# Prologue and first two slots of an attention and two-layer MLP kernel, each engine's calls written out one by one, without filler matmuls

## The reference, cut to what matters

```
q_d, k_d, v_d = mean of q, k, v over groups of 4 positions     # batch 4, heads 8, 576 positions, head dim 64
out_d   = softmax(q_d k_d^T / 8) v_d                           # 144 x 144 per head
out_up  = repeat(out_d, 4)
local   = softmax(where(|i - j| < 4, q k^T / 8, -1e9)) v
x  = (out_up + local), 2304 tokens x 512
x  = (max(x @ w_in1, 0)) ** 2 @ w_out1                         # 512 -> 2048 -> 512
x  = softplus(x @ w_in2) @ w_out2
```

## Time and profile before

| | us |
|---|---|
| median of 3 runs | 907.18 |
| the runs | 907.07, 907.18, 908.58 |
| profiled execution, its own time | 908.52 |
| its span, first to last instruction | 906.7 |
| TensorE busy | 887.1 (98%) |
| VectorE, ScalarE, GpSimd busy | 612.5, 440.0, 331.4 |
| granted clock of TensorE, mean | 0.992 |

### The profile page before, as it was taken

The page is one execution under the profiler, slowest core; times in us unless marked ns, Lnnn a source line. Parts: engine busy times, 40 slices in busy tenths (PEclk is TensorE's granted clock), DMA queues, the critical chain, the costliest instruction groups (busy, mean ns, idle before and its releaser), DMA issues.

```text
span 906.7 us, 14878 instructions
## 1 busy us (share of the span) xinstructions
PE 887.1 (98%) x5765; PEld 831.7 (92%) x5765; DVE 612.5 (68%) x1058; ACT 440.0 (49%) x1073; POOL 331.4 (37%) x160
## 2 busy tenths in 40 slices
PE   9889899999999999999999999999999999999998
PEld 7678799999999999999999998999989999899997
DVE  3779767866765776645145977767767777677675
ACT  4766354544546445453466634434444434434433
POOL 8699868688585976856100000000000000000000
PEclk9899999999999999999999999999999999999999
DMA  9770231221424221100145300200200200200000
GB/s 300 258 288 25 70 137 60 86 98 65 151 71 137 85 71 42 45 27 1 57 153 168 118 1 1 70 1 1 70 1 1 71 0 1 70 1 1 36 1 35
DMA packets 22037, 65.14 MB, mean 72 GB/s; under 512 B 2272, under 2 KB 9440, under 8 KB 21968
## 3 DMA queue, kind: packets, MB, share of 16 engines
q1 hardware_dynamic: 21968, 64.20, 21.0%
HBM read 54.76 MB, written 9.44 MB: 71 GB/s over the span
## 4 chain that ended last, share of the span: by engine, by line
PE 88%; POOL 6%; issue 2%; DVE 2%; ACT 1%; DMA 0%; POOLq 0%; DVEq 0%
PE bank L1285 22%; PE bank L1299 22%; PE bank L696 20%; PE bank L647 20%; POOL w_lo L725 2%; POOL prod L451 2%; POOL prod L405 1%; PE bank L545 1%; PE bank L288 1%; PE bank L590 1%; PE bank L472 1%; PE bank L615 1%; DMA qk_first<-in_qk_grp 0%; DVE xs L482 0%; ACT bank L565 0%
## 5 line engine op out<-in xcount | busy, mean ns | idle before, releaser
L647 PE MATMUL bank<-x_hi,w_hi 128*128 128x288 f32 x508 | 155.9, 307 | 3.9 <-DVE g_lo L685 2.1
L451 POOL TENSOR_TENSOR prod<-sc,vt 128x1344 f32<-128x1344 f32 x42 | 134.9, 3233 | 61.0 <-DVE sc L439 53.5
L685 DVE TENSOR_TENSOR g_lo<-bank,g_hi 128x288 fp32r<-128x288 f32 x128 | 58.4, 456 | 144.0 <-ACT g_hi L680 143.9
L696 PE MATMUL bank<-g_hi,w_hi 128*128 128x288 f32 x512 | 151.3, 295 | 0.0
L696 PE MATMUL bank<-g_hi,w_lo 128*128 128x288 f32 x512 | 151.1, 295 | 0.0
L696 PE MATMUL bank<-g_lo,w_hi 128*128 128x288 f32 x512 | 151.0, 295 | 0.0
L647 PE MATMUL bank<-x_lo,w_hi 128*128 128x288 f32 x508 | 150.9, 297 | 0.0
L647 PE MATMUL bank<-x_hi,w_lo 128*128 128x288 f32 x508 | 150.8, 297 | 0.0
L1011 ACT ACTIVATE sp_abs<-bank 128x384 f32<-128x384 f32 x96 | 47.0, 490 | 194.4 <-PE bank L1285 194.3
L405 POOL TENSOR_TENSOR prod<-qt,kt 128x1344 f32<-128x1344 f32 x42 | 133.1, 3175 | 17.9 <-DVE sc L412 12.3
L1285 PE MATMUL bank<-x_lo,w_hi 128*128 128x384 f32 x384 | 129.9, 338 | 0.0
(11 more groups left out here) (110 smaller groups left out, 1620.3 us busy)
## 6 DMA issues: line engine op xcount, KB each, us to landing
w_raw<-in_w SPq DMA_DIRECT2D x32, 512.0 KB, 4.8
qk<-in_qk_grp SPq DMA_DIRECT2D x12, 576.0 KB, 4.9
kt<-in_k_loc SPq DMA_DIRECT2D x7, 960.0 KB, 4.9
vt<-in_v_loc SPq DMA_DIRECT2D x7, 960.0 KB, 4.8
vg<-in_v_grp SPq DMA_DIRECT2D x16, 320.0 KB, 3.5
x_scratch<-ys SPq DMA_DIRECT2D x32, 144.0 KB, 3.2
x_raw<-x_scratch SPq DMA_DIRECT2D x6, 768.0 KB, 4.6
out<-y SPq DMA_DIRECT2D x18, 256.0 KB, 2.0
```

What stands on the lines that cost most here:

```text
L451: nc.gpsimd.tensor_tensor(dst, pb, win, ALU.mult).then_inc(prod_ready[m % 2], 1)
L647: last = nc.tensor.matmul(h_ps[f % 2][:, 0:NT], w[:, f, wc], x[:, T % 2, kc], start=(kc == 0 and i == 0), stop=(kc == KC - 1 and i == 2))
L685: nc.vector.tensor_tensor(g_lo[:, f % 2], h_ps[f % 2][:, 0:NT], g_hi[:, f % 2].bitcast(F32), ALU.subtract).then_inc(g_ready, 1)
L696: last = nc.tensor.matmul(y_ps[d][:, 0:NT], w[:, f, wc], g[:, f % 2], start=(f == 0 and i == 0), stop=(f == FC - 1 and i == 2))
```

## The change

It replaces the prologue's lists and the loops over slots 0 and 1 by lists of single calls, for all five queues. The calls are the same, with these exceptions and moves:

- all `keep_busy` calls are gone (the helper is redefined and no longer called; `first_x` loses its argument);
- SyncE: `first_load(1)` goes to second place, `v0` from second place to after `w_raw` 0 and slot 1's q and k; `w_raw` 0 goes ahead of slot 1's q and k; later loads are interleaved with the pair loads otherwise;
- GpSimd: the pools are interleaved otherwise, `weight_lo(0)` stands before the first `score_mult`, `first_pool_v(3)` after the third;
- ScalarE: `weight_hi(0)` after `first_exp(1)`, `weight_hi(1)` before `first_split_hi(1)`; `pair_exp` waits for `up_ready` for odd n above 4;
- VectorE: `score_sum(1, 0)` and `(1, 1)` before the last `first_split_lo`, `(1, 3)` before slot 0; in the slots the order is new throughout;
- TensorE: `pair_turn(0)` before `first_scores(2)`, `first_hidden_in` 0 and 1 before `first_x(2)`, and the attention's calls at other steps;
- waits on `mask_done` in `first_pool` and `first_pool_v`, since the mask is now a helper of its own (`local_mask`, the same calls, at the same place in the list).

The core of the diff (indentation cut by eight; slot 1, where the order of the same calls changes likewise, and what stood in the loops is left out):

```diff
     pool.wait_ge(first_qk[j], 16)
     if j:
         pool.wait_ge(qk0_pooled, j)
+        pool.wait_ge(mask_done, 1)
     two = qk_first[:, j].rearrange("p s (g f) -> p (s g) f", f=2)
     half = pairs0[:].rearrange("p s g -> p (s g)")
     nc.gpsimd.tensor_tensor(half, two[:, :, 0], two[:, :, 1], ALU.add).then_inc(pairs0_ready, 1)
...
 def first_pool_v(pool, j):
     pool.wait_ge(first_vg[j], 16)
+    pool.wait_ge(mask_done, 1)
     if j:
         pool.wait_ge(v0_pooled, j)
     two = vg0[0:GH, j].rearrange("g m (t f) -> g (m t) f", f=2)
...
 def keep_busy(pe, times):
     for _ in range(times):
-        nc.tensor.matmul(X0[:, 0:P], ident[:], ident[:], start=True, stop=True)
+        nc.tensor.matmul(t_ps[P - 32:P, 0:P], ident[:, P - 32:P], ident[:], start=True, stop=True)
 def first_scores(pe, j):
     pe.wait_ge(first_qk[j], 16)
...
     for e in range(2):
         nc.vector.tensor_copy(pT0[0:BK, j % 2, e], first_banks(j)[e][0:BK, 0:NT]).then_inc(pT0_copied, 1)
-def first_x(pe, j, busy):
+def first_x(pe, j):
     if j:
         pe.wait_ge(x0_ready, j)
         pe.wait_ge(up_ready, j)
-    keep_busy(pe, busy)
     if j == 0:
         pe.wait_ge(v0_loaded, 16)
     pe.wait_ge(pT0_copied, 2 * j + 2)
...
     a.wait_ge(ds_max, 2 * n + 2)
     if n:
         a.wait_ge(dp_ready, 2 * n)
+    if n > KC and n % 2:
+        a.wait_ge(up_ready, n)
     nc.scalar.activation(dnb[:], dmx[:], ACT.Copy, scale=-SCALE / (FACTOR * FACTOR)).then_inc(dnb_ready, 1)
     a.wait_ge(dnb_ready, n + 1)
     for e in range(2):
...
     def load_x2(i):
         sp.dma_start(x2_raw[:], x2_dram[:, :, i * NT2:i * NT2 + NT2]).then_inc(x2_loaded, 16)
+    def first_load_v0():
+        sp.dma_start(v0[0:BKR], v_first).then_inc(v0_loaded, 16)
+    def first_room_free():
+        sp.wait_ge(x0_ready, KC)
+        sp.wait_ge(up_ready, KC)
     first_load(0)
-    sp.dma_start(v0[0:BKR], v_first).then_inc(v0_loaded, 16)
+    first_load(1)
     first_load_v(0)
-    first_load(1)
     first_load(2)
+    first_load(3)
     first_load_v(1)
-    first_load(3)
     first_load_v(2)
+    weight_load(sp, 0, w1)
+    local_load_qk(1)
+    first_load_v0()
+    weight_load(sp, 1, w1)
+    weight_load(sp, 2, w1)
+    weight_load(sp, 3, w1)
+    weight_load(sp, 4, w1)
     first_load_v(3)
-    local_load_qk(1)
-    for f in range(3):
-        weight_load(sp, f, w1)
-    pair_load_qk(KC)
-    pair_load_v(KC)
-    for f in range(3, 5):
-        weight_load(sp, f, w1)
+    pair_load_qk(4)
+    weight_load(sp, 5, w1)
+    weight_load(sp, 6, w1)
+    weight_load(sp, 7, w1)
+    pair_load_v(4)
     local_load_v(1)
-    for f in range(5, LATE):
-        weight_load(sp, f, w1)
     pair_load_qk(5)
+    weight_load(sp, 8, w1)
+    first_room_free()
+    weight_load(sp, 9, w1)
+    weight_load(sp, 10, w1)
+    weight_load(sp, 11, w1)
+    weight_load(sp, 12, w1)
+    pair_load_qk(6)
+    weight_load(sp, 13, w1)
     pair_load_v(5)
-    sp.wait_ge(x0_ready, KC)
-    sp.wait_ge(up_ready, KC)
-    for f in range(LATE, FC):
-        weight_load(sp, f, w1)
-    pair_load_qk(6)
+    weight_load(sp, 14, w1)
     local_load_qk(2)
     pair_load_v(6)
+    weight_load(sp, 15, w1)
     local_load_v(2)
+    output_store(0)
     pair_load_qk(7)
-    for T in range(1, TILES):
+    pair_load_v(7)
+    local_load_qk(3)
+    pair_load_qk(8)
+    pair_load_v(8)
+    pair_load_qk(9)
+    local_load_v(3)
+    for T in range(2, TILES):
         C, A_next = 2 * T + 5, 2 * T + 6
-        if T == 1:
-            output_store(0)
+        if A_next < KC * B:
+            pair_load_qk(A_next)
+        if C < KC * B:
             pair_load_v(C)
-            pair_load_qk(A_next)
-            local_load_qk(3)
-        else:
-            if A_next < KC * B:
-                pair_load_qk(A_next)
-            if C < KC * B:
-                pair_load_v(C)
-            if T == TILES - 1:
-                sp.wait_ge(x_ready, KC * (TILES - 1))
-                sp.wait_ge(ys_stored, 16 * KC * (TILES - 2))
-                load_x2(0)
-            output_store(T - 1)
+        if T == TILES - 1:
+            sp.wait_ge(x_ready, KC * (TILES - 1))
+            sp.wait_ge(ys_stored, 16 * KC * 2)
+            load_x2(0)
+        output_store(T - 1)
         if T == 2:
             local_load_qk(4)
         if A_next < KC * B:
...
+    local_mask(pool)
     first_pool(pool, 1)
     first_pool_v(pool, 0)
+    first_pool(pool, 2)
     first_pool_v(pool, 1)
-    first_pool(pool, 2)
+    first_pool(pool, 3)
+    weight_lo(pool, 0, 0, w_lo_pool)
     first_pool_v(pool, 2)
-    first_pool_v(pool, 3)
-    first_pool(pool, 3)
     score_mult(pool, 1, 0)
     score_mult(pool, 1, 1)
-    def lo(f):
-        weight_lo(pool, f, 0, w_lo_pool)
-    lo(0)
-    lo(1)
     score_mult(pool, 1, 2)
-    lo(2)
+    first_pool_v(pool, 3)
     score_mult(pool, 1, 3)
-    lo(3)
+    weight_lo(pool, 1, 0, w_lo_pool)
+    weight_lo(pool, 2, 0, w_lo_pool)
+    weight_lo(pool, 3, 0, w_lo_pool)
     score_mult(pool, 1, 4)
-    lo(5)
     score_mult(pool, 1, 5)
-    lo(7)
-    lo(9)
+    weight_lo(pool, 5, 0, w_lo_pool)
+    weight_lo(pool, 7, 0, w_lo_pool)
+    weight_lo(pool, 9, 0, w_lo_pool)
     value_mult(pool, 1, 0)
     value_mult(pool, 1, 1)
-    lo(11)
+    weight_lo(pool, 11, 0, w_lo_pool)
     value_mult(pool, 1, 2)
     value_mult(pool, 1, 3)
-    lo(13)
     value_mult(pool, 1, 4)
+    weight_lo(pool, 13, 0, w_lo_pool)
     value_mult(pool, 1, 5)
-    lo(15)
-    for T in range(TILES - 1):
-        x_at = min(2 * T + 2, NPROD) if T < 2 else 5 if T == 2 else NPROD
+    weight_lo(pool, 15, 0, w_lo_pool)
+    score_mult(pool, 2, 0)
+    score_mult(pool, 2, 1)
+    x_split_lo(pool, 1)
+    score_mult(pool, 2, 2)
+    score_mult(pool, 2, 3)
+    score_mult(pool, 2, 4)
+    score_mult(pool, 2, 5)
+    value_mult(pool, 2, 0)
+    value_mult(pool, 2, 1)
+    value_mult(pool, 2, 2)
+    value_mult(pool, 2, 3)
+    value_mult(pool, 2, 4)
+    value_mult(pool, 2, 5)
+    score_mult(pool, 3, 0)
+    score_mult(pool, 3, 1)
+    score_mult(pool, 3, 2)
+    score_mult(pool, 3, 3)
+    x_split_lo(pool, 2)
+    score_mult(pool, 3, 4)
+    score_mult(pool, 3, 5)
+    value_mult(pool, 3, 0)
+    value_mult(pool, 3, 1)
+    value_mult(pool, 3, 2)
+    value_mult(pool, 3, 3)
+    value_mult(pool, 3, 4)
+    value_mult(pool, 3, 5)
...
-    first_masks(a)
-    first_exp(a, 0)
-    pair_exp(a, 0)
-    first_exp(a, 1)
-    pair_exp(a, 1)
-    first_exp(a, 2)
-    pair_turn_copy(a, 1)
-    first_split_hi(a, 0)
-    pair_exp(a, 2)
-    first_exp(a, 3)
-    pair_turn_copy(a, 2)
-    first_split_hi(a, 1)
-    pair_exp(a, 3)
-    weight_hi(a, 0, 0)
-    first_split_hi(a, 2)
-    pair_turn_copy(a, 3)
-    weight_hi(a, 1, 0)
-    first_split_hi(a, 3)
-    weight_hi(a, 2, 0)
-    weight_hi(a, 3, 0)
-    weight_hi(a, 4, 0)
-    hidden_act(a, 0, 0)
...
+    first_masks(a)
+    first_exp(a, 0)
+    pair_exp(a, 0)
+    first_exp(a, 1)
+    weight_hi(a, 0, 0)
+    pair_exp(a, 1)
+    first_exp(a, 2)
+    pair_turn_copy(a, 1)
+    pair_exp(a, 2)
+    first_split_hi(a, 0)
+    first_exp(a, 3)
+    weight_hi(a, 1, 0)
+    first_split_hi(a, 1)
+    pair_turn_copy(a, 2)
+    pair_exp(a, 3)
+    first_split_hi(a, 2)
+    weight_hi(a, 2, 0)
+    pair_turn_copy(a, 3)
+    weight_hi(a, 3, 0)
+    weight_hi(a, 4, 0)
+    first_split_hi(a, 3)
+    weight_hi(a, 5, 0)
+    hidden_act(a, 0, 0)
+    weight_hi(a, 6, 0)
+    hidden_act(a, 0, 1)
+    hidden_act(a, 0, 2)
+    pair_exp(a, 4)
+    hidden_act(a, 0, 3)
+    hidden_act(a, 0, 4)
+    weight_hi(a, 7, 0)
+    weight_hi(a, 8, 0)
+    softmax_exp(a, 1)
+    weight_hi(a, 9, 0)
+    weight_hi(a, 10, 0)
+    hidden_act(a, 0, 5)
+    spread_up(a, 1)
+    pair_turn_copy(a, 4)
+    hidden_act(a, 0, 6)
+    weight_hi(a, 11, 0)
+    weight_hi(a, 12, 0)
+    weight_hi(a, 13, 0)
+    hidden_act(a, 0, 7)
+    hidden_act(a, 0, 8)
+    pair_exp(a, 5)
+    hidden_act(a, 0, 9)
+    hidden_act(a, 0, 10)
+    hidden_act(a, 0, 11)
+    weight_hi(a, 14, 0)
+    pair_turn_copy(a, 5)
+    weight_hi(a, 15, 0)
+    hidden_act(a, 0, 12)
+    hidden_act(a, 0, 13)
+    hidden_act(a, 0, 14)
+    x_split_hi(a, 1)
+    hidden_act(a, 0, 15)
+    hidden_act(a, 1, 0)
+    pair_exp(a, 6)
+    output_copy(a, 0)
...
+    first_max(dve, 0)
+    pair_max(dve, 0)
+    first_norm(dve, 0)
+    first_max(dve, 1)
+    pair_norm(dve, 0)
+    first_turn_copy(dve, 0)
+    pair_turn_copy0(dve)
+    first_norm(dve, 1)
+    pair_max(dve, 1)
+    first_max(dve, 2)
+    first_turn_copy(dve, 1)
+    pair_norm(dve, 1)
+    first_max(dve, 3)
+    first_norm(dve, 2)
+    pair_max(dve, 2)
+    pair_norm(dve, 2)
+    first_split_lo(dve, 0)
+    pair_up(dve, 0)
+    score_sum(dve, 1, 0)
+    first_norm(dve, 3)
+    first_split_lo(dve, 1)
+    pair_max(dve, 3)
+    first_turn_copy(dve, 2)
+    pair_up(dve, 1)
+    score_sum(dve, 1, 1)
+    pair_norm(dve, 3)
+    first_split_lo(dve, 2)
+    pair_up(dve, 2)
+    first_turn_copy(dve, 3)
+    pool_qk(dve, 4)
+    score_sum(dve, 1, 2)
```

(161 more changed lines are left out.)

175 lines of the change are left out of this document (87 added, 88 removed).

## The result

| | before | after |
|---|---|---|
| median of 9 runs, us | 907.48 (907.07 to 908.58) | 910.25 (908.99 to 912.04) |
| profiled execution, its own time | 908.52 | 908.99 |
| its span | 906.7 | 907.2 |

The change makes the kernel slower: the ratio is 1.0028, with a 95% interval from 1.0017 to 1.0039. The median lies 1.8 us above the top of the range, and the forecast of 902.4 was on the wrong side.

A forecast was written before the change was run, and what follows sets the result against it. Only work before slot 1's first group could gain, with GpSimd setting the leg: prologue end 48.5 + leg 59.5 = 108.0 us against 112.8, 4.8 less, so a median of 902.4; range 894.0 to 908.5.

The forecast's parts named there:

- The prologue of the change: Step pricing the five new prologue lists at both TensorE clocks; it chose a prologue end of 48.5 us, 4.0 later.
- P: End of the prologue, at first_hidden_in(..., last=True): 44.5 us before, forecast 48.5, with a range from 46 to 51.
- the walk: Hand pricing of the new prologue lists, step by step: end at 40.9 us at 2.4 GHz, 52.6 at 1.2 GHz.
- the leg: From the prologue's end to the end of hidden_in(1, 0), slot 1's first group: forecast 59.5 us, before 68.3.
- The fillers: Prologue, TensorE: much of their 12.54 us was waiting time anyway; without them nothing occupies TensorE before 5.3 us.
- The softmax: Slot 0, the softmax that value_mult(1, 0) waits for: ready 21 us after P, before 24.9.
- The rest: End of the leg: two score_mult 6.2 us, x_split_lo 3.1, and 0.4 for the last matmuls.
- Slot 1: TensorE's holes of before are 0.35 + 0.23 us, so nothing is won; a possible small loss is hidden.
- Low clock throughout: Rival: prologue at 1.2 GHz, P = 52.6, gain 0.7 us, time 906.5; chance 0.15.
- Full clock soon: Rival: prologue at 2.4 GHz, P = 40.9, gain 12.4 us, time 894.8; chance 0.13.
- The low clock sets everything: Rival: P at its upper bound of 62.4, 9.1 us more, time 916.3; sign P past 53.3; chance 0.05.

The follow-up runs named there:

- x6: The changed kernel with 49 fillers in all holes of the prologue, all narrow (32 columns of weights); 896.21 us, ratio to before 0.9878.
- x1: The kernel before with its 35 fillers left out, nothing else changed; 912.81 us, ratio to before 1.0061.
- x4: The kernel before with the new prologue's lists put in, without fillers, and the old loops over slots 0 and 1; 910.87 us, ratio to before 1.0044.
- x8: The changed kernel with weight_hi(0), weight_hi(1) and weight_lo(0) put back where the kernel before has them; 920.81 us, ratio to before 1.0141.
- x5: The changed kernel with 49 fillers, 29 of full width and 20 narrow ones in the later holes; 896.94 us, ratio to before 0.9887.
- x9: The changed kernel with 42 narrow fillers in the prologue's holes, none ahead of the first scores; 896.39 us, ratio to before 0.9881.

## Why the prediction was wrong

**The step that failed** is the choice in "The prologue of the change": "I take 1.2 GHz to about 28 us and 2.4 GHz after", P = 48.5. The ground I gave was that unbroken work from 23 us would raise the clock. TensorE did have that work, stretch after stretch with 2.00 of 2.00 us busy, and the clock stayed at 0.50 to 56 us: P came at 53.46, 5.0 us later than forecast. The two ends of the walk were good. At 1.2 GHz throughout it gave P = 52.6, measured 53.46. At 2.4 GHz it gave 40.9; in x6 the last four matmuls begin at 40.53 and last 0.68, 41.2. I had both numbers, and chose between them on a rule about TensorE being busy which my own rows had only partly borne out: the earlier trace rows show 9.5 us of nearly unbroken work at 1.2 GHz.

From the forecast of 902.4 to the measured 910.25 the steps are: 5.0 us of P, 2.1 of the leg, 1.8 back in slot 1, and 2.5 between the profiled executions and the medians, of which 2.3 no profile shows and 0.3 is the median of before (907.18, later 907.48).

**The fillers.** I said that much of their 12.54 us was waiting time anyway, and that their loss would cost through the clock. Both hold: x1 is 6.0 us slower without them. But I put P 4.0 us later than before, and it was 8.7 to 8.9 later.

**The leg**, forecast 59.5, measured 61.6. The softmax, forecast 21 us after P, came at 21.1. Six `value_mult` and three `weight_lo` were to take 28.8 us and took 105.1 - 74.6 = 30.5, `weight_lo(11)` alone 4.27 instead of 2.4. (The terms as I wrote them make 29.1, not 28.8.) The rest, 10.0 us, is within 0.3 of the 9.7 forecast. x4 shows that the prologue's lists carry the leg's gain. That `weight_lo(0)` in GpSimd's idle time is part of it is my account of the leg; x8, which moves it together with two `weight_hi`, doesn't show it by itself.

**Slot 1**: I forecast nothing and it gave 1.8 us, in every pair of kernels that differ in it (792.1 to 792.2 against 793.9 to 794.0). I had read TensorE's holes off its busy time, and the timeline of the kernel before shows what that mostly hides:

```profile
...
168.64 0.40 PE L647 MATMUL bank<-x_hi,w_hi 128*128 128x288 f32 x1
...
169.39 0.40 PE L647 MATMUL bank<-x_hi,w_hi 128*128 128x288 f32 x1
...
170.15 0.40 PE L647 MATMUL bank<-x_hi,w_hi 128*128 128x288 f32 x1
...
```

The last three quarters of `hidden_in(2, 0)` begin 0.75 us apart, each waiting for its piece of `x_split_lo`, which begins at 167.03; three matmuls back to back take 0.40. That is 1.05 us, of which only some 0.23 shows as idle time, since the records overlap; it is the hole that the earlier trace rows have behind 168 us. With the 0.35 ahead of 168 it makes 1.4 of the 1.8; the other 0.4 stays open. The new list has that `x_split_lo` at 166.39, though it entered the slot 2.25 us later.

**The rivals.** "Low clock throughout" was the case that came true (0.15), with 906.5 for it; P was 0.9 later and the leg 2.1 longer than it assumed, slot 1 1.8 shorter, which gives 907.7 for the median. The measured 910.25 is 2.5 above that, the last of the steps above. "Full clock soon", 894.8, is what x5, x6 and x9 made real, at 896.2 to 896.9. "The low clock sets everything", with P at 62.4 by counting half of all throttled time as lost, is not what happened, though P at 53.46 did pass the 53.3 that I had named as its sign: 53.46 - 40.9 = 12.6 of the 21.5 us were on the chain. As I cited it, that rule of the Trainium skill (TensorE: Matmul & The Clock Gate, "HAM oscillation") gives an upper bound here, 21.5 us against the 12.6; in this prologue TensorE shares the chain with ScalarE and VectorE.

## What to carry to other kernels

When fillers are taken away, price the prologue at both clocks and don't assume that useful work will bring the clock up by itself: here nearly the whole of the prologue ran at 1.2 GHz. The new order with small fillers in all its holes is 10 to 11 us faster than the kernel before; without them it is 2.8 us slower. Put small fillers into every hole of TensorE's list, sized by the times at full clock, the late ones above all: x6 and x9 are 1.2% faster than the kernel before. And look for what shortens a stage in the lists ahead of it too: behind the new prologue the leg is 60.9 to 63.8 us (x8 left out), behind the old one 67.8 to 69.2, with either order of slot 0. Which of the calls done ahead carries it is open.

## What the hardware showed that was not expected

- TensorE stayed at a granted clock of 0.50 from 14 to 56 us with 37 of these 42 us busy, mostly on small fp32 matmuls and transposes; the clock rose once the 128x288 matmuls of slot 0 ran. Yet the first 4 us of the same kind of work, from 4.6 to 8.8, had brought it up, and in x9 too; in x4, with the same calls, it did not (the mask's two matmuls at 9.10 take 0.82). What sets these apart no run here shows.
- Behind 14 records of 32 columns of weights in 3.00 us (x6) `first_scores` takes 0.77, as behind 14 of 128 columns in 3.35 (x5); behind the same 14 wide ones in the earlier trace rows it takes 1.34.
- The profile's granted clock reads 1.00 from the start even where the durations are those of 1.2 GHz (x1, x4), until the first change is recorded.
- `weight_lo` on VectorE takes from 1.2 to 4.2 us, and 10.37 once in x8, with GpSimd busy throughout; in the changed kernel GpSimd's own goes from 2.35 to 4.27 us beside VectorE's work.
